# Pad lanes left out of the scatters, and two scatters of a block under way together, in an attention and mixture-of-experts kernel

## The chip, the cores and the metric

One core of one Trainium2 chip. The time is the device time of one execution in microseconds (us); lower is better. One execution was profiled. Its own time stands beside its span, which runs from the first to the last instruction.

## What is computed

The reference first computes attention with 4 batches, 8 heads, 576 positions and head size 64, with a bias on the scores made by a small network over relative positions. The result, read as 2304 rows of 512, is the input x of a mixture of 8 experts:

```python
logits = x @ w_gate
noise_scale = np.log1p(np.exp(x @ w_noise))
noisy_logits = logits + noise_scale * noise
top2 = np.argpartition(-noisy_logits, 2, axis=1)[:, :2]
...
out = np.zeros((N, D), dtype=np.float32)
for e in range(E):
    for k in range(2):
        mask = top2[:, k] == e
        h = np.maximum(x[mask] @ w1[e], 0.0)
        out[mask] += top2_w[mask, k, None] * (h @ w2[e])
```

Each row goes to two experts, so 4608 row visits are shared out. With the reference's inputs the experts get 616, 594, 556, 539, 534, 562, 609 and 598 of them.

## The kernel before, in words

**Stages.** The first stage, about 340 us, is the attention. During it the rows of x are stored to an HBM tensor (`xs`), and 128 pad rows of zeros are put behind them (L1592). The routing then makes lists of row numbers (`rowi`), one column per tile. The second stage is the experts.

**Blocks and tiles.** A block is up to 620 rows of one expert: 5 tiles (`BT`) of 124 rows (`ROWS`) each. A tile of indices has 128 lanes, and the lanes that hold no row of the expert hold a pad index, 2304 (`N`) or more, different in each lane. Here 8 blocks run, one for each expert: block 0 is written out by hand, then a hardware loop of 3 pairs of blocks, then a last block. The parity i says which of two sets of buffers a block uses (1 for odd blocks).

**One block.** POOL (GpSimd) gathers the rows of x by index into `xg` (L1620), ahead by one to two blocks, and the routing weights of the rows into `wrow` (L1625). PE transposes the rows (`xtr`, L773 to L780), ACT and DVE make a high and a low part of them (L1500, `xlow` L1258), and PE multiplies by the first weights (`first`, L782) and the second (`second`, L789), each in three passes. The second product of a tile lands in one of two banks `po`. DVE (in block 0 also ACT, `scaled0` at L1455 to L1458) multiplies it by the routing weight into one of two buffers `ys` (L1291, L1122). POOL then issues a scatter: an indirect DMA that adds the 128 rows of `ys` to the rows of the output that the indices name (L1633). A pad lane adds its row into one of 128 spare rows behind the output. The output was zeroed during the attention.

**What orders the work around the change.** One semaphore, `y_added`, counts the landings of the scatters and of the store of the pad rows, 16 for each DMA (`C_ADD` is the store's part). Waiting on it are:
- POOL in `scatter` (L1630): scatter g is issued once all g earlier ones have landed, and once its `ys` is there (L1631).
- POOL at the top of `block_of` (L1644), before it copies the block's indices into `iscat`, which the scatters read.
- DVE before it writes `ys` (L1290, L1121), and ACT before the third tile of block 0 (L1523): the scatter that read this buffer two tiles ago must have landed.
- POOL before the first gathers (L1667), for the store of the pad rows, and SP at the end (L565).

POOL works through its list in order. In block 0 that is: gathers of tiles 3 and 4, scatter 0, two weight gathers, scatter 1, the gathers of block 1 (tiles 0 to 2), scatter 2, tiles 3 and 4, one gather of block 2, scatter 3, two gathers, scatter 4, two gathers (L1680 to L1700). In a later block it is: index copies, five weight gathers, then gather and scatter in turn for tiles 0 to 2, two scatters, two gathers (L1642 to L1663). SP loads the expert weights in pieces of 512 KB into `wraw` (L506 to L512). ACT and DVE split each piece into a high and a low part (L1371, L989) in an order written out with their other work. For block 1 this is at L1296 to L1307: the last four splits, then `scaled0(3)`, then `xlow` of tiles 5 to 7.

Of the kernel before, what the change touches and what calls it, by code (L numbers as in the profile page):

```python
# [24 lines left out]
P = 128  # L25
# [4 lines left out]
N, DM, NE, F = B * S, H * D, 8, 1024  # L30
# [20 lines left out]
BT = 5  # L51
# [117 lines left out]
def build(nc, qT, kT, v, rtab, pcol, rcp8, w1c, b1c, w2b, wg, noise, mw1, mw2, consts, out, xs):  # L169
    ctx = ExitStack()  # L170
    with ctx:
# [3 lines left out]
        def sem(name):  # L175
            return ctx.enter_context(nc.semaphore(name))
# [33 lines left out]
        zeros = tmp("zeros", [P, DM])  # L210
# [209 lines left out]
        y_done = sem("y_done")  # L420
        y_added = sem("y_added")
        icopied = sem("icopied")
# [12 lines left out]
        def piece_rows(g, i, bank):  # L435
# [4 lines left out]
                    bank[0:XT, 0:len(cs) * 4 * D].rearrange("p (c e) -> p c e", c=len(cs)))  # L440

        CONSTS = 16 * (2 * GQ + 2)
        CONSTS2 = 16 * 3

        C_XLO, C_HLO, C_Y, C_ADD = 2, 4, 2, 16

# [8 lines left out]
        def _(sp):  # L455
# [103 lines left out]
            pairs = sp.value_load(blocks[0:1, NBLK:NBLK + 1], min_val=NE // 2 - 1, max_val=NBLK // 2 - 1)  # L559
            with sp.Fori(0, pairs) as k:  # L560
                for i in range(2):
                    e = expert(2 * k + 2 + i)
                    sp.wait_ge(y_ready, BT * (2 * k + i + 1))
                    load_expert(i, e)
            sp.wait_ge(y_added, C_ADD + 16 * BT * (2 * pairs + 2))  # L565
            sp.sem_inc(sp_passed, 1)
# [347 lines left out]
        def _(dve):  # L914
# [140 lines left out]
            for t in range(TILES):  # L1055
# [14 lines left out]
                b, at = divmod(t - 1 - GLAG - (H - 1) * NU, H * NU)  # L1070
# [47 lines left out]
            def scaled0(t):  # L1118
                dve.wait_ge(y_ready, t + 1)
                dve.wait_ge(w_rows, 16 * BT)  # L1120
                dve.wait_ge(y_added, C_ADD + 16 * (t - 1))  # L1121
                V.tensor_scalar(ys[t % 2][:, :], po[:, t % 2, :], wrow[:, t, 0:1], None, ALU.mult).then_inc(y_done, 1)  # L1122
# [146 lines left out]

            def block_of(b, i, last):  # L1270
                e = dve.value_load(blocks[0:1, bass.ds(b, 1)], min_val=0, max_val=NE - 1)
                for n in range(C_HALVES):
                    half, f = divmod(n, CF)
                    cols = slice(half * HB, (half + 1) * HB)
                    dve.wait_ge(hhi_done, C_HALVES * b + n + 1)
                    V.scalar_tensor_tensor(out=hC[1][:, f, cols], in0=ps[n % 4 // 2][:, n % 2, 0:HB], scalar=0.0,  # L1276
                                           in1=hC[0][:, f, cols].bitcast(F32), op0=ALU.max, op1=ALU.subtract)\
                        .then_inc(hlo_done, 1)
                    if n in XLATE:
                        t = XLATE[n]  # L1280
                        xlow(BT * b + t, (i + t) % 2, t)
                for t in range(BT):
                    g = BT * b + t
                    if not last and 2 * t < NC:
                        for c in (2 * t, 2 * t + 1):
                            split(b + 1, 1 - i, c, c)
                    dve.wait_ge(y_ready, g + 1)
                    if t == 0:
                        dve.wait_ge(w_rows, 16 * BT * (b + 1))
                    dve.wait_ge(y_added, C_ADD + 16 * (g - 1))  # L1290
                    V.tensor_scalar(ys[(i + t) % 2][:, :], po[:, (i + t) % 2, :], wrow[:, t, bass.ds(e, 1)], None, ALU.mult)\  # L1291
                        .then_inc(y_done, 1)
                    if not last and t < XB:
                        xlow(g + BT, (i + 1 + t) % 2, t)
# [14 lines left out]
            with dve.Fori(0, pairs) as k:  # L1309
                block_of(2 * k + 1, 1, False)  # L1310
                block_of(2 * k + 2, 0, False)
            block_of(2 * pairs + 1, 1, True)


        @block.scalar
        def _(act):
# [205 lines left out]
            xcopy(4, 0, 4)  # L1522
            act.wait_ge(y_added, C_ADD + 16)  # L1523
            scaled0(2)
# [18 lines left out]
        def _(pool):  # L1543
# [37 lines left out]
            def list_constants():  # L1581
# [9 lines left out]
                nc.gpsimd.memset(rowi[:, NL:NL + BT], N).then_inc(consts_done, 1)  # L1591
                pool.dma_start(xs[N:N + P, :], zeros[:, :]).then_inc(y_added, 16)  # L1592

# [7 lines left out]
            for n in range(B * H):  # L1601
                ahead = n + 2 < B * H
# [26 lines left out]
            def scatter(g, index, i):  # L1629
                pool.wait_ge(y_added, C_ADD + 16 * g)  # L1630
                pool.wait_ge(y_done, C_Y + g + 1)  # L1631
                pool.sem_inc(pool_passed, 1)
                nc.gpsimd.indirect_dma_start(out=out, out_offset=bass.IndirectOffsetOnAxis(ap=index, axis=0),  # L1633
                                             in_=ys[i][:, :], in_offset=None, compute_op=ALU.add,
                                             bounds_check=N + P - 1, oob_is_err=True).then_inc(y_added, 16)

# [4 lines left out]

            def block_of(b, i, ahead):  # L1642

                pool.wait_ge(y_added, C_ADD + 16 * BT * b)  # L1644
                pool.sem_inc(pool_passed, 1)
# [19 lines left out]
            for half in range(2):  # L1665
                pool.wait_ge(x_stored[half], 16 * (B - 1))
            pool.wait_ge(y_added, C_ADD)  # L1667
            pool.wait_ge(consts_done, 6)
# [34 lines left out]
            with pool.Fori(0, pairs) as k:  # L1703
                block_of(2 * k + 1, 1, True)
                block_of(2 * k + 2, 0, True)
            block_of(2 * pairs + 1, 1, False)


# [53 lines left out]
```

## Time and profile before

| | before |
|---|---|
| median of 3 runs | 798.24 us (796.75 to 800.86) |
| the profiled execution | 798.18 us, span 796.0 us, mean granted TensorE clock 0.988 |
| busy: PE (matmul) | 759.8 us, 95% of the span |
| busy: DVE, ACT, POOL | 492.2, 393.1, 383.2 us |
| software DMA queue (POOL's) | 10720 packets, 22.72 MB |
| the scatters in POOL's time | 40, about 1.6 us each |

How to read it: PE, DVE, ACT, POOL and SP are the engines TensorE, VectorE, ScalarE, GpSimd and SyncE; PEld is PE's weight load. L784 is line 784 of the kernel. The busy time of a DMA that POOL issues is the time in which POOL writes its descriptors, not the transfer. The chain is followed back from the last instruction, at each step to what released it. Releasers are inferred from semaphore events, so the engine named in a row can be the wrong one where the wait was for several things.

### The profile page before, as it was taken

How to read it: one execution, taken by the hardware profiler on the slowest of the kernel's cores; microseconds unless marked ns; L12 is line 12 of the kernel's file. 1: busy time of each engine (PE TensorE's matmuls, PEld its weight loads, DVE VectorE, ACT ScalarE, POOL GpSimd, SP SyncE). 2: the span in 40 equal slices, each digit the busy share in tenths (PEclk: the TensorE clock that was granted, in tenths of full speed). 3: DMA queues.
4: the chain of work that ended last, by engine and by line, in shares of the span. 5: the costliest groups of instructions: out<-in, count | busy, mean ns of one | idle time of the engine just before them, and what ended most of it. 6: DMA issues, size and time to landing. Idle time of an engine off the chain costs nothing.

```text
span 796.0 us, 18523 instructions
## 1 busy us (share of the span) xinstructions
PE 759.8 (95%) x6658; PEld 615.2 (77%) x6658; DVE 492.2 (62%) x1228; ACT 393.1 (49%) x843; POOL 383.2 (48%) x440
## 2 busy tenths in 40 slices
PE   4887999999999998999999999999999999999995
PEld 2335676776776765979898998998998988988984
DVE  6897999998999897886436235235344344354311
ACT  5996888888888786505334133233232232232200
POOL 0008999899899784035434324324424413423412
PEclk9998999999999999999999999999999999999998
DMA  7776343353353363319633724714804805713213
GB/s 165 211 232 150 112 134 104 103 164 103 100 166 99 95 203 148 86 26 297 194 137 66 203 77 75 234 35 79 264 6 76 263 12 81 251 26 66 41 19 48
DMA packets 51719, 98.49 MB, mean 124 GB/s; under 512 B 12736, under 2 KB 21696, under 8 KB 51648
## 3 DMA queue, kind: packets, MB, share of 16 engines
q1 hardware_dynamic: 40352, 74.55, 30.4%
q0 software_dynamic: 10720, 22.72, 14.5%
q8 instruction: 43, 0.70, 0.4%
q10 hardware_dynamic: 576, 0.29, 0.2%
q14 instruction: 28, 0.23, 0.1%
HBM read 66.38 MB, written 20.53 MB: 109 GB/s over the span
## 4 chain that ended last, share of the span: by engine, by line
PE 82%; DMA 6%; ACT 4%; DVE 3%; issue 3%; POOL 0%; POOLq 0%; SPq 0%; DVEq 0%; ACTq 0%
PE ps L784 26%; PE po L801 24%; PE po L696 11%; PE ps L614 8%; PE pt L641 6%; DMA slab<-work 2%; DMA out_rows<-ys,iscat 2%; PE pt L620 2%; ACT work L1331 2%; ACT work L1350 2%; PE pt L655 1%; PE pt L628 1%; DMA b1col<-in_b1c 1%; DVE ns L957 0%; DVE hT L1114 0%
## 5 line engine op out<-in xcount | busy, mean ns | idle before, releaser
L801 PE MATMUL po<-whi,hT 128*128 128x512 f32 (+1 forms) x640 | 162.7, 399 | 0.1
L784 PE MATMUL ps<-xT,whi 128*128 128x310 f32 (+1 forms) x960 | 160.0, 305 | 0.0
L1512 ACT ACTIVATE hT<-ps 128x310 fp32r<-128x310 f32 x112 | 48.2, 430 | 199.1 <-PE ps L784 199.1
L784 PEld LDWEIGHTS ps<-xT,whi 128*128 128x128 f32 x960 | 142.4, 189 | 0.9
L801 PEld LDWEIGHTS po<-whi,hT 128*128 128x128 f32 (+1 forms) x640 | 119.0, 189 | 26.0 <-DVE hT L1114 0.5
L1276 DVE SCALAR_TENSOR_TENSOR hT<-ps,hT 128x310 fp32r<-128x310 f32 x112 | 53.8, 481 | 133.2 <-ACT hT L1512 133.2
L1578 POOL TENSOR_SCALAR work<-work,rcp 128x576 f32<-128x576 f32 (+1 forms) x160 | 117.6, 745 | 25.6 <-DVE rcp L970 25.1
L1366 ACT ACTIVATE work<-ns,nmax 128x576 f32<-128x576 f32 (+1 forms) x160 | 123.1, 770 | 4.3 <-DVE nmax L957 4.2
L957 DVE CUSTOM_DVE_ANT_0 ns<-ps,slab 128x576 f32<-128x576 f32 (+1 forms) x160 | 119.7, 750 | 8.2 <-PE ps L614 6.4
L1620 POOL DMA_INDIRECT xg<-x_rows,igath x38 | 43.0, 1132 | 159.8 <-DVE ys L1291 74.2
L1633 POOL DMA_INDIRECT out_rows<-ys,iscat x35 | 60.3, 1724 | 95.1 <-DMA out_rows<-ys,iscat 65.1
L696 PE MATMUL po<-work,vs 128*64 128x288 f32 x640 | 98.2, 421 | 0.7 <-DVE xnat L985 0.7
L1291 DVE TENSOR_SCALAR ys<-po,wrow 128x512 f32<-128x512 f32 x35 | 26.3, 751 | 98.8 <-PE po L801 98.8
L784 PE MATMUL ps<-xT,wlo 128*128 128x310 f32 (+1 forms) x480 | 86.5, 302 | 0.0
L989 DVE TENSOR_TENSOR wlo<-wraw,whi 128x1024 fp32r<-128x1024 f32 x64 | 76.0, 1222 | 14.0 <-ACT whi L1371 14.0
L1381 ACT ACTIVATE work<-pt 128x320 f32<-128x320 f32 x144 | 62.9, 437 | 37.5 <-PE pt L641 30.6
L801 PE MATMUL po<-wlo,hT 128*128 128x512 f32 (+1 forms) x320 | 80.6, 394 | 0.0
L641 PEld LDWEIGHTS pt<-cst,work 64*128 64x128 f32 x1280 | 52.8, 141 | 35.1 <-POOL work L1578 19.4
L784 PEld LDWEIGHTS ps<-xT,wlo 128*128 128x128 f32 x480 | 72.8, 188 | 0.0
L801 PEld LDWEIGHTS po<-wlo,hT 128*128 128x128 f32 (+1 forms) x320 | 60.0, 188 | 14.2
L978 DVE COPY work<-pt 128x320 f32<-128x320 f32 x133 | 64.9, 488 | 9.9 <-PE pt L641 4.4
L641 PE MATMUL pt<-cst,work 64*128 64x64 f32 x1280 | 66.9, 231 | 2.8 <-DVE work L978 1.3
(181 smaller groups left out, 1109.0 us busy)
## 6 DMA issues: line engine op xcount, KB each, us to landing
wraw<-in_mw SPq DMA_DIRECT2D x64, 512.0 KB, 9.8
slab<-work SPq DMA_DIRECT2D x36, 288.0 KB, 3.7
qraw<-in_qT SPq DMA_DIRECT2D x64, 144.0 KB, 2.8
vs<-in_v SPq DMA_DIRECT2D x32, 160.0 KB, 2.5
out_rows<-zeros SPq DMA_DIRECT2D x32, 152.0 KB
kraw<-in_kT SPq DMA_DIRECT2D x64, 72.0 KB, 2.3
x_rows<-xnat SPq DMA_DIRECT2D x8, 576.0 KB, 4.3
xg<-x_rows,igath POOLq DMA_INDIRECT x38, 3.5
```

The costliest lines, as they stand in the source:

```text
L614: mm = nc.tensor.matmul(ps[t % 2][:, half, 0:HALF], qq[n % 2][part(half), u * P:(u + 1) * P], kk[n % 2][part(half), :], start=i == 0, stop ...
L641: mm = nc.tensor.transpose(pt[half][:, kt * D:(kt + 1) * D], E[t % ER][part(half), kt * P:(kt + 1) * P], ident[part(half), part(half)])
L696: mm = nc.tensor.matmul(po[half * D:(half + 1) * D, n % 2, 0:HALF], vs[n % 4][:, kt, :], PT[n % 2][:, kt, half * HALF:(half + 1) * HALF], ...
L784: mm = nc.tensor.matmul(ps[n % 4 // 2][:, n % 2, 0:w], w1s[i][pw][:, c, f * P:(f + 1) * P], x[px][:, c, :], start=j == 0 and c == 0, stop= ...
L801: mm = nc.tensor.matmul(po[0:m, (i + t) % 2, :], hT[px][:, at:at + m], w2s[i][pw][:, c, :], start=j == 0 and c == 0, stop=j == 2 and c == ...
L957: nc.vector.tensor_tensor_reduce(out=ns[t % 2][0:r, :].rearrange("p (a s) -> p a s", a=2), in0=ps[t % 2][0:r, :, 0:HALF], in1=bias[0:r, u, ...
L978: nc.vector.tensor_copy(PT[n % 2][:, :, u * P:u * P + D], pt[0][:, 0:NU * D].rearrange("p (k s) -> p k s", k=NU))\
L989: nc.vector.tensor_tensor(wlo[i][:, c * WC:(c + 1) * WC], wraw[i][:, c * WC:(c + 1) * WC], whi[i][:, c * WC:(c + 1) * WC].bitcast(F32), AL ...
L1366: nc.scalar.activation(E[t % ER][0:r, 0:S], ns[t % 2][0:r, :], ACT.Exp, bias=nmax[0:r, i:i + 1], scale=-1.0, accum_out=ssum[0:r, i:i + 1]) ...
L1381: nc.scalar.activation(PT[n % 2][:, :, at:at + D], pt[1][:, 0:NU * D].rearrange("p (k s) -> p k s", k=NU), ACT.Copy).then_inc(t_done[1], 1)
L1578: nc.gpsimd.tensor_scalar(E[t % ER][0:r, 0:S], E[t % ER][0:r, 0:S], rcp[0:r, i:i + 1], 1.0, ALU.mult, ALU.mult)\
L1633: nc.gpsimd.indirect_dma_start(out=out, out_offset=bass.IndirectOffsetOnAxis(ap=index, axis=0), in_=ys[i][:, :], in_offset=None, compute_o ...
```

## The change

Three things. The scatter's index check has the bound N - 1 in place of N + P - 1 and no longer counts an index beyond it as an error, so the lanes with pad indices are left out. `y_added` becomes two semaphores, one for each `ys` buffer (even and odd tiles), and the store of the pad rows gets its own. And `scatter` no longer waits for the earlier scatters: the wait before writing `ys` is for the last scatter of the same parity, and the top of `block_of` on POOL waits for all scatters of the block before, by two waits. `added(k, i, t)` gives 16 times the number of earlier tiles of the same parity.

```diff
-        y_added = sem("y_added")
+        y_added = [sem(f"y_added{i}") for i in range(2)]
+        xpad_stored = sem("xpad_stored")
...
+        def added(k, i, t):
+
+            return 16 * (BT * k + (BT * (2 - i) + t) // 2)
...
-            sp.wait_ge(y_added, C_ADD + 16 * BT * (2 * pairs + 2))
+            sp.wait_ge(y_added[0], 16 * BT * (pairs + 1))
+            sp.wait_ge(y_added[1], 16 * BT * (pairs + 1))
...
             def scaled0(t):
                 dve.wait_ge(y_ready, t + 1)
                 dve.wait_ge(w_rows, 16 * BT)
-                dve.wait_ge(y_added, C_ADD + 16 * (t - 1))
+                dve.wait_ge(y_added[t % 2], 16 * (t // 2))
...
-            def block_of(b, i, last):
+            def block_of(k, i, last):
+                b = 2 * k + 2 - i
...
-                    dve.wait_ge(y_added, C_ADD + 16 * (g - 1))
+                    dve.wait_ge(y_added[(i + t) % 2], added(k, i, t))
...
-            act.wait_ge(y_added, C_ADD + 16)
+            act.wait_ge(y_added[0], 16)
...
-                pool.dma_start(xs[N:N + P, :], zeros[:, :]).then_inc(y_added, 16)
+                pool.dma_start(xs[N:N + P, :], zeros[:, :]).then_inc(xpad_stored, 16)
...
             def scatter(g, index, i):
-                pool.wait_ge(y_added, C_ADD + 16 * g)
                 pool.wait_ge(y_done, C_Y + g + 1)
                 pool.sem_inc(pool_passed, 1)
                 nc.gpsimd.indirect_dma_start(out=out, out_offset=bass.IndirectOffsetOnAxis(ap=index, axis=0),
                                              in_=ys[i][:, :], in_offset=None, compute_op=ALU.add,
-                                             bounds_check=N + P - 1, oob_is_err=True).then_inc(y_added, 16)
+                                             bounds_check=N - 1, oob_is_err=False).then_inc(y_added[i], 16)
...
-            def block_of(b, i, ahead):
-
-                pool.wait_ge(y_added, C_ADD + 16 * BT * b)
+            def block_of(k, i, ahead):
+                b = 2 * k + 2 - i
+                for t in range(2):
+                    pool.wait_ge(y_added[(i + t) % 2], added(k, i, t))
...
-            pool.wait_ge(y_added, C_ADD)
+            pool.wait_ge(xpad_stored, 16)
```

The calls of `block_of` pass k in place of the block's number on DVE and POOL.

## Rows read from the trace of the kernel before

**Rows 1.** The page's part 4: shares of the chain by engine.

```profile
PE 82%; DMA 6%; ACT 4%; DVE 3%; issue 3%; POOL 0%; POOLq 0%; SPq 0%; DVEq 0%; ACTq 0%
```

**Rows 2.** Waits of PE from 335 us to the end: us in total, times, longest.

```profile
PE pt L620 <- issue: 2.0, 1, 2.0
PE pt L620 <- DMA xg<-x_rows,rowi: 0.3, 1, 0.3
```

**Rows 3.** The chain in order of time, 550 to 800 us: start, us, what.

```profile
702.66 5.57 PE po L801 x24
...
759.97 5.58 PE po L801 x24
...
765.88 0.76 DVE ys L1291
...
767.55 4.69 DMA out_rows<-ys,iscat
...
778.66 4.65 DMA out_rows<-ys,iscat
...
784.24 4.83 DMA out_rows<-ys,iscat
```

**Rows 4.** Timeline of the end: start, us, engine, line, operation, idle before.

```profile
788.06 0.75 DVE L1291 TENSOR_SCALAR ys<-po,wrow 128x512 f32<-128x512 f32 x1 [4.81 <-PE po L801]
790.00 1.55 POOL L1633 DMA_INDIRECT out_rows<-ys,iscat  x1 [4.21 <-DMA out_rows<-ys,iscat]
```

**Rows 5.** Windows at the end: busy time by engine, PE clock, DMA share, GB/s.

```profile
791.50:792.00 0.50, 0.00 (x0) 0.00 (x0) 0.00 (x0) 0.00 (x0) 0.06 (x1) 0.50 0.00 0
792.00:792.50 0.50, 0.00 (x0) 0.00 (x0) 0.00 (x0) 0.00 (x0) 0.00 (x0) 0.50 1.17 86
...
794.00:794.50 0.50, 0.00 (x0) 0.00 (x0) 0.00 (x0) 0.00 (x0) 0.00 (x0) 0.50 0.17 25
```

**Rows 6.** Waits of POOL from 596 to 653 us, one block.

```profile
POOL out_rows L1633 <- DMA out_rows<-ys,iscat: 8.2, 2, 4.3
```

**Rows 7.** Timeline of POOL in block 0.

```profile
360.14 1.02 POOL L1625 DMA_INDIRECT wrow<-w_rows,rowi  x1 [0.31 <-issue]
362.63 1.61 POOL L1633 DMA_INDIRECT out_rows<-ys,rowi  x1 [1.47 <-ACT ys L1458]
...
373.00 1.61 POOL L1633 DMA_INDIRECT out_rows<-ys,rowi  x1 [4.72 <-DMA out_rows<-ys,rowi]
```

**Rows 8.** Timeline of ACT in block 0.

```profile
351.07 0.69 ACT L1458 ACTIVATE ys<-po,wrow 128x512 f32<-128x512 f32 x1 [1.64 <-PE po L801]
...
361.72 0.69 ACT L1458 ACTIVATE ys<-po,wrow 128x512 f32<-128x512 f32 x1 [1.35 <-DMA wrow<-w_rows,rowi]
```

**Rows 9.** Timeline of all engines around PE's wait, 376 to 388 us.

```profile
377.86 2.11 PE L801 MATMUL po<-whi,hT 128*128 128x512 f32 x8
...
380.14 1.06 ACT L1371 ACTIVATE whi<-wraw 128x1024 fp32r<-128x1024 f32 x1 [1.07 <-DMA wraw<-in_mw]
...
381.24 1.23 DVE L989 TENSOR_TENSOR wlo<-wraw,whi 128x1024 fp32r<-128x1024 f32 x1 [0.90 <-ACT whi L1371]
...
383.04 1.25 DVE L1261 TENSOR_TENSOR xT<-pt,xT 128x496 fp32r<-128x496 f32 x2
...
383.81 0.61 PE L620 MATMUL pt<-cst,xg 124*128 124x124 f32 x4 [1.99 <-issue]
...
384.18 3.66 PE L801 MATMUL po<-whi,hT 128*128 128x512 f32 x8
```

**Rows 10.** Windows around the same wait; columns as in rows 5.

```profile
372.00:380.00 8.00, 8.00 (x40) 6.59 (x39) 4.91 (x5) 4.08 (x5) 5.50 (x5) 1.00 0.96 335
380.00:384.00 4.00, 2.01 (x10) 1.35 (x9) 3.10 (x5) 2.00 (x3) 1.24 (x1) 1.00 0.27 74
384.00:388.00 4.00, 4.00 (x15) 3.25 (x14) 1.09 (x3) 0.58 (x1) 3.36 (x3) 0.57 0.48 65
```

**Rows 11.** The scatters in POOL's time: ns, least, median and most.

```profile
L1633 POOL DMA_INDIRECT out_rows<-ys,iscat x35: 1552/1622/2159, 424.3 to 790.0; - x35
```

More of the change, by code:

```diff
@@ L440, in piece_rows @@
                     bank[0:XT, 0:len(cs) * 4 * D].rearrange("p (c e) -> p c e", c=len(cs)))
+        def added(k, i, t):
+            return 16 * (BT * k + (BT * (2 - i) + t) // 2)
         CONSTS = 16 * (2 * GQ + 2)
         CONSTS2 = 16 * 3
-        C_XLO, C_HLO, C_Y, C_ADD = 2, 4, 2, 16
+        C_XLO, C_HLO, C_Y = 2, 4, 2
         xw = nc.dram_tensor("w_rows", (N + P, NE), F32, kind="Internal").ap()
@@ L1309, in _ @@
             with dve.Fori(0, pairs) as k:
-                block_of(2 * k + 1, 1, False)
-                block_of(2 * k + 2, 0, False)
-            block_of(2 * pairs + 1, 1, True)
+                block_of(k, 1, False)
+                block_of(k, 0, False)
+            block_of(pairs, 1, True)
         @block.scalar
@@ L1703, in _ @@
             with pool.Fori(0, pairs) as k:
-                block_of(2 * k + 1, 1, True)
-                block_of(2 * k + 2, 0, True)
-            block_of(2 * pairs + 1, 1, False)
+                block_of(k, 1, True)
+                block_of(k, 0, True)
+            block_of(pairs, 1, False)
 def kernel(**inputs):
```

## The prediction

> **What bounds the kernel now.** I read the page's chain first, then the waits of TensorE, then the end of the chain in order of time, then the stretch in which the first scatters run. The page gives PE 82% of the chain and DMA 6% [rows 1]. In the list of waits from 335 us on, PE waits twice in 461 us: 2.0 us before a transpose of gathered rows, and 0.3 us [rows 2]. So from block 1 on PE runs without a gap, and a scatter can only matter where it holds that one wait of 2.0 us or stands behind PE's last instruction. In the last block the chain leaves PE at 765.55 and passes from scatter to scatter, each 4.5 to 4.8 us under way [rows 3]. That looks like a scatter-bound tail, but PE makes a tile in 5.57 us, and a scatter with its 0.93 us of queue steps takes 5.5 to 5.8 us: the two run level. What counts is the last tile. DVE ends the scaled rows of tile 4 at 788.06 + 0.75 = 788.81; the last scatter starts at 790.00 and waited for the one before, which had started at 784.24 and taken 4.83 us [rows 3, 4]. Its rows move between 792.0 and about 794.1, and the span ends at 796.0 [rows 5].
>
> **Part one: two scatters under way.** Before, scatter g waited for all earlier ones; now the landing is waited for by the engine that overwrites its buffer (ys), two tiles later, and by the next block's first scatter.
>
> Last scatter. Tile 0 of the last block shows the delay when nothing is under way: ys ends at 765.88 + 0.76 = 766.64, the scatter starts at 767.55, so 0.91 us [rows 3]. Tile 4 would start at 788.81 + 0.91 = 789.72 in place of 790.00: a gain of 0.28 us. All of it lies on the path that sets the end. ys of tile 4 itself needs scatter 2, landed at 778.66 + 4.65 = 783.31 [rows 3], which is long past.
>
> The six blocks in the middle. POOL loses waits of about 4 us before the scatters of tiles 3 and 4 (8.2 us in two waits in one block [rows 6]). They are worth nothing: PE has no wait there [rows 2]. The cover is the 57.3 us of PE work per block (702.66 to 759.97 [rows 3]). The fifth scatter of a block still waits for its own ys, so the copy of the next block's indices, behind all landings, moves by some tenths. The DVE wait is one against one, with a computed value in both versions.
>
> The first block. Scatter 0 had landed at about 361.70: ACT's ys of tile 2, which waits for that landing, starts at 361.72, and scatter 1 starts 0.93 us after it, at 362.63. The row names ACT ys as releaser, yet by the code scatter 1 needs ys of tile 1, which was done at 351.8; it was the landing [rows 7, 8]. Now scatter 1 can follow the weight gather that ends at 360.14 + 1.02 = 361.16, some 0.3 us later, at 361.46: 1.17 us earlier. Scatter 2 waited 4.72 us for scatter 1 [rows 7] and goes at about 368.6 in place of 373.00, and the two gathers queued behind it on POOL go some 4 us earlier too. Who gains? PE's wait of 2.0 us ends with DVE's subtraction for tile 5 (started 383.04). Before it in DVE's order stand ys of tile 3 and the last of the weight splits (381.24), which hangs on ACT (380.14), which waited 1.07 us for an expert weight load [rows 9]. So PE waits for the weight loads, and no scatter is in that chain except as a rival for the DMA engines. These are full: share 0.96 from 372 to 380, then 0.27 [rows 10]. Full engines do the same work in whatever order. Everything that I move ahead was also moved before 380 in the old order, so the last load ends when it did, less what the earlier start uses of free time before 363. The start is 1.17 us earlier, at the edge of the full stretch; I take 0.2 us off the wait, between 1.2 (the whole shift) and minus 4 (below, second rival).
>
> **Part two: pad lanes left out.** A tile has 124 real lanes of 128. The last tile of a block has fewer: the reference's inputs give the last expert 598 rows, so the last scatter carries 598 - 496 = 102 lanes, and 26 are left out. Its transfer takes 2.1 us [rows 5]. If time goes by bytes, that is 2.1 x 26/128 = 0.43 us less; if the engine with the most lanes decides and keeps its 8, nothing. Dealt round, the fullest engine would carry 7 lanes in place of 8: 0.26 us. I take 0.2, and both ends go into the range. The rows show the 16 engines evenly busy (share 1.17 falling to 0.17 in the last half microsecond), which tells nothing of how lanes are dealt. The Trainium skill ("DMA: Bandwidth & Descriptors", The descriptor swizzle) says that each engine carries eight fixed lanes in two runs of four, such as 64 to 67 and 96 to 99; lanes 102 to 127 would then leave some engines with all eight, and by it this term is 0 and my sum 0.2 us smaller. For other blocks the saved bytes (4 lanes a tile, up to 82 more in a last tile) are hidden behind PE.
>
> Leaving a lane out also changes what POOL does when it writes a scatter's descriptors: 1.55 to 2.16 us now [rows 11]. No row shows that form. Nearest are the scatters themselves; the cost lies between 0.6 less (one spread of these rows) and 0.6 more, and I take 0. It would count once, at the last scatter.
>
> **Small things.** The index copy waits for two semaphores in place of one, and so does SP at the end: all queue steps between ys and scatter together take 0.91 us [rows 3], so one more of them is put at 0.05 us on the path. The pad store has a semaphore of its own, with the same waiter.
>
> **Sum.** -0.28 (last scatter) -0.2 (lanes) -0.2 (PE's wait) +0.05 = -0.63 us. The profiled execution took 798.18 us (span 796.0 and 2.18 around it), so 797.55. The median of the runs shown, 798.24, stands 0.06 above it: 797.6.
>
> **The rivals.**
> One: PE's wait goes away. If the queue of scatters was slowing the weight loads more than by bytes, the last load lands 2 us earlier. Then PE gains the 2.0 us, and also the slow matmuls behind it: eight took 3.66 us after the pause, in a stretch whose granted clock was 0.57, near the 1.2 GHz level; eight of the same kind had taken 2.11 us before it [rows 9, 10]. That is 1.6 us more. With the tail's 0.43 it makes -4.0: 794.2, right at the edge of 0.5%. Against: full engines, and only 24 KB of pads left out of these three scatters. Chance 0.07, faster by over 0.5% in most of it.
> Two: the opposite. Scatter 2 and two gathers enter the queue earlier and push the loads back. Were none of these three served before the last load until now, they would cost it a scatter (about 2 us of transfer) and two gathers of about half that each: 4 us. PE's wait grows to 6.0 us: 798.2 + 4.0 - 0.43 = 801.8 at worst, and 799 to 800 for a part. Against: share 0.27 after 380 means that they were done by then. Chance 0.11, nearly all of it inside 0.5%.
> Three, on the other side: generating a scatter that may leave lanes out is much slower on POOL. Place: the tail, where scatter work and PE are level at 5.57 us. A scatter takes 1.55 + 0.9 us of POOL's time, so up to 3.1 us more fit into a tile's time, and only the last one's own excess counts. From there each tile adds to a lag. At 4.65 us more (four times now) POOL would take 7.1 us a tile: 4 x 1.5 + 4.65 = 10.7 later, 808.3 with the rest of the sum. It decides from about 3.4 us more on. For it: nothing in the rows shows the form. Against: the index check is there before as well. Chance 0.03.
> Four: leaving a lane out does not shorten anything, since each costs a descriptor all the same: -0.4, 797.8. Chance 0.24; it can hardly be told from the forecast.
>
> **How the numbers follow.** The forecast keeps 0.55. Everything but rivals one and three and the worst of two lies within 0.5% (4.0 us), about what a measurement of this kernel can tell from no change. Faster 0.06, same 0.90, slower 0.04. The range: unknown costs down (0.23 more by lanes, 0.6 by generation, 1.0 by the wait) give 795.8, up (rival two in part, 0.6 generation) about 800.5; the runs before spread by 4 us themselves. I give 795.3 to 800.6.
>
> **What would show it.** The last scatter starts 0.9 us after its ys and not after the landing before it. The wait of PE near 382 is 1.8 us. Scatter 1 starts near 361.5, scatter 2 near 368.6. No PE wait in the middle. Packets of the software queue fall by about 500 if a lane left out is not sent. I am wrong if PE's wait moves by over 1 us, if a scatter holds POOL for over 3 us, or if any block takes other than 57.3 us.

## The result, and the profile after

| | before | after |
|---|---|---|
| median of 12 runs | 797.68 us (795.86 to 800.86) | 800.12 us (796.73 to 803.70) |
| ratio, 95% interval | | 1.0034 [1.0020, 1.0048] |
| profiled execution | 798.18 us, span 796.0 | 800.05 us, span 798.2 |
| mean granted clock | 0.988 | 0.986 |

The changed kernel is slower, by 0.34% or 2.7 us (1.6 to 3.8). The forecast was 0.6 us faster; the time lies inside the range of 795.3 to 800.6, on the wrong side of no change.

The page's parts 2 to 4 of the changed kernel: packets in all, the software queue, shares of the chain by engine.

```profile
DMA packets 51720, 97.44 MB, mean 122 GB/s; under 512 B 13249, under 2 KB 22209, under 8 KB 51649
...
q0 software_dynamic: 10720, 21.67, 14.3%
...
PE 87%; ACT 3%; DMA 3%; DVE 3%; issue 2%; SPq 0%; POOLq 0%; POOL 0%; ACTq 0%; DVEq 0%
```

Against [rows 1] PE's share of the chain rose from 82% to 87% and DMA's fell from 6% to 3%: the scatters that stood in it one behind the other have left the chain, as meant. The queue still handles 10720 packets, for 1.05 MB less.

**The end.** The last tile in the changed kernel's timeline (to compare with [rows 4]), and the windows in which its rows move (to compare with [rows 5]).

```profile
790.45 0.75 DVE L1298 TENSOR_SCALAR ys<-po,wrow 128x512 f32<-128x512 f32 x1 [4.70 <-PE po L807]
...
792.07 1.55 POOL L1639 DMA_INDIRECT out_rows<-ys,iscat  x1 [3.90 <-DVE ys L1298]
```

```profile
793.50:794.00 0.50, 0.00 (x0) 0.00 (x0) 0.00 (x0) 0.00 (x0) 0.12 (x1) 0.50 0.00 0
794.00:794.50 0.50, 0.00 (x0) 0.00 (x0) 0.00 (x0) 0.00 (x0) 0.00 (x0) 0.50 1.22 66
...
796.00:796.50 0.50, 0.00 (x0) 0.00 (x0) 0.00 (x0) 0.00 (x0) 0.00 (x0) 0.50 0.25 41
```

The scatter starts 792.07 - 791.20 = 0.87 us after its rows are scaled, and what it waited for is DVE, not the landing. The rows still move for over 2 us, at 66 GB/s in the first window where it was 86. From issue to the end of the span it is 6.1 us, 6.0 before: 26 lanes fewer shortened nothing.

**The first block.** POOL's timeline (to compare with [rows 7]):

```profile
361.97 1.02 POOL L1632 DMA_INDIRECT wrow<-w_rows,rowi  x1 [0.31 <-issue]
363.29 1.61 POOL L1639 DMA_INDIRECT out_rows<-ys,rowi  x1 [0.30 <-issue]
366.80 1.07 POOL L1627 DMA_INDIRECT xg<-x_rows,rowi  x1 [1.90 <-DVE rowi L1098]
...
371.95 1.62 POOL L1639 DMA_INDIRECT out_rows<-ys,rowi  x1 [0.30 <-issue]
373.88 1.07 POOL L1627 DMA_INDIRECT xg<-x_rows,rowi  x1 [0.30 <-issue]
375.25 1.78 POOL L1627 DMA_INDIRECT xg<-x_rows,rowi  x1 [0.31 <-issue]
```

All of this block lies later on the clock than before, so the tables below count from one mark that the change doesn't reach, PE's transpose of tile 3: 357.60 before, 359.49 after. Counted so, scatter 1 starts at 3.80 in place of 5.03, and scatter 2 at 12.46 in place of 15.40, 2.9 us earlier, with its two gathers behind it. The forecast had scatter 2 4.4 us earlier; part of that was taken up by the gathers ahead of it, which end later than forecast. Now the wait of PE (to compare with [rows 9, 10]).

```profile
382.63 1.06 ACT L1378 ACTIVATE whi<-wraw 128x1024 fp32r<-128x1024 f32 x1 [1.42 <-DMA wraw<-in_mw]
...
383.73 1.23 DVE L995 TENSOR_TENSOR wlo<-wraw,whi 128x1024 fp32r<-128x1024 f32 x1 [1.25 <-ACT whi L1378]
...
386.30 0.61 PE L626 MATMUL pt<-cst,xg 124*128 124x124 f32 x4 [2.65 <-issue]
...
386.67 3.49 PE L807 MATMUL po<-whi,hT 128*128 128x512 f32 x8
```

```profile
376.00:380.00 4.00, 4.00 (x24) 3.35 (x23) 2.35 (x3) 1.75 (x2) 1.99 (x2) 1.00 1.06 342
380.00:382.00 2.00, 2.00 (x10) 1.64 (x9) 0.99 (x2) 1.06 (x1) 1.04 (x1) 1.00 0.64 258
...
386.70:390.10 3.40, 3.40 (x11) 2.68 (x10) 0.75 (x2) 0.58 (x1) 2.79 (x3) 0.54 0.43 39
```

The chain is the one the prediction read: a load of 512 KB, ACT's part, DVE's part, DVE's subtraction, PE. But the last load is used at 382.63 - 359.49 = 23.14 from the mark, where it was 380.14 - 357.60 = 22.54, and PE's wait grew from 1.99 to 2.65 us.

**The blocks between** (chain in order of time, to compare with the first lines of [rows 3]):

```profile
647.84 5.57 PE po L807 x24
...
705.16 5.57 PE po L807 x24
...
762.47 27.85 PE po L807 x120
```

57.32 and 57.31 us a block, as before. In the last block the chain stays with PE for all five tiles (120 matmuls), where it had left PE after the first.

So one profile of each kernel gives +1.9 us ahead of the mark, +0.6 from the mark to block 1's start (35.21 and 35.82) and -0.3 from there to the end: with one execution of each that settles nothing, as the spread over the runs below shows.

### The profile page after: what moved, and what is told of

It is laid out like the page before. It is cut to its first block, busy times and chain, and to the rows that moved or that the text cites. A ratio compares the mean times of both kernels' runs of the same rounds, so it can differ in the third digit from the quotient of the medians.

```text
span 798.2 us, 18492 instructions
## 1 busy us (share of the span) xinstructions
PE 762.2 (95%) x6658; PEld 617.5 (77%) x6658; DVE 491.8 (62%) x1228; ACT 393.8 (49%) x843; POOL 387.6 (49%) x440
## 3 DMA queue, kind: packets, MB, share of 16 engines
q0 software_dynamic: 10720, 21.67, 14.3%
## 4 chain that ended last, share of the span: by engine, by line
PE 87%; ACT 3%; DMA 3%; DVE 3%; issue 2%; SPq 0%; POOLq 0%; POOL 0%; ACTq 0%; DVEq 0%
PE po L807 28%; PE ps L790 26%; PE po L702 11%; PE ps L620 8%; PE pt L647 6%; DMA slab<-work 3%; PE pt L626 2%; ACT work L1338 2%; ACT work L1357 1%; PE pt L661 1%; PE pt L634 1%; DMA b1col<-in_b1c 1%; DVE wlo L995 1%; PE ps L596 1%; DVE hT L1120 0%
## 5 line engine op out<-in xcount | busy, mean ns | idle before, releaser
L1627 POOL DMA_INDIRECT xg<-x_rows,igath x38 | 41.3, 1087 | 178.3 <-DVE ys L1298 125.6
L1639 POOL DMA_INDIRECT out_rows<-ys,iscat x35 | 63.9, 1826 | 81.1 <-DVE ys L1298 75.2
L702 PE MATMUL po<-work,vs 128*64 128x288 f32 x640 | 100.2, 428 | 0.7 <-DVE xnat L991 0.7
L995 DVE TENSOR_TENSOR wlo<-wraw,whi 128x1024 fp32r<-128x1024 f32 x64 | 76.1, 1222 | 14.1 <-ACT whi L1378 11.4
```

Of the source, the lines that this page charges most:

```text
L702: mm = nc.tensor.matmul(po[half * D:(half + 1) * D, n % 2, 0:HALF], vs[n % 4][:, kt, :], PT[n % 2][:, kt, half * HALF:(half + 1) * HALF], ...
L995: nc.vector.tensor_tensor(wlo[i][:, c * WC:(c + 1) * WC], wraw[i][:, c * WC:(c + 1) * WC], whi[i][:, c * WC:(c + 1) * WC].bitcast(F32), AL ...
```

## The experiments

**Theories.** *Order of the transfers:* in block 0 the wait for scatter 1 had kept scatter 2 and two gathers back, so that they moved behind the weight loads; now they move ahead of them, the last load lands later and PE waits (the prediction's rival two). *DVE stopped by POOL:* in the changed kernel DVE stands still while POOL writes scatter 1's descriptors, and that delays the splits. *Lanes:* leaving lanes out costs something by itself. *Later blocks:* two scatters under way there disturb PE or its loads. The expectations were written before each set of runs and name the theories as they stood then: theory 1 and theory Q are the order of the transfers, theory 2 is the lanes, theory 3 is something outside the scatters, such as the attention stage or the program's code, and theory P is the stop of DVE.

All diffs are against the changed kernel, unless the kernel before is named. Ratios are against the kernel before on the same chip.

### First four: the parts alone

The lanes alone, on the kernel before (it still waits for every landing):

```diff
-                                             bounds_check=N + P - 1, oob_is_err=True).then_inc(y_added, 16)
+                                             bounds_check=N - 1, oob_is_err=False).then_inc(y_added, 16)
```

> Before's waits and its one semaphore, with only the index bound changed so that pad lanes are left out. Theory 1 (the loss comes from scatters of block 0 that enter the DMA queue earlier and hold back the weight loads): nothing of the order changes, so 0 to -0.4 us against before (797.3 to 797.7), and PE's wait near 382 us stays at about 2.0 us. Theory 2 (leaving lanes out is itself dearer, in descriptor writing or in transfer): the whole +2.4 us is here, about 800. Theory 3 (the loss has nothing to do with scatters, but with how the program's code or timing falls in the attention stage and in instruction fetches): the time differs from before by anything up to 2 us and the difference shows ahead of 340 us.

Block 0 one at a time, later blocks as changed (the five calls in block 0 pass `True`):

```diff
-            def scatter(g, index, i):
+            def scatter(g, index, i, serial=False):
+                if serial and g:
+                    pool.wait_ge(y_added[1 - i], 16 * ((g + 1) // 2))
```

> The changed kernel, but in block 0 each scatter again waits for the one before it; later blocks keep two under way, lanes are left out. Theory 1: the loss goes away, about 797.3, PE's wait back at 2.0 us, and DVE does not stop for 2 us before the last list of rows. Theories 2 and 3: stays at about 800.

Block 0 as changed, later blocks one at a time:

```diff
             def block_of(k, i, ahead):
...
+                    pool.wait_ge(y_added[(i + t + 1) % 2], 16 * (BT * k + (BT * (2 - i) + t + 1) // 2))
```

> The changed kernel, but in all blocks after block 0 each scatter again waits for the one before it. Theory 1: stays slow, about 800.4 (0.3 us of the last scatter given back). Theory 3: anything. If the time falls to about 798, the loss was in the later blocks, where neither profile shows a wait of PE.

And the changed kernel unaltered, as a repeat:

> The changed kernel once more, unaltered, for a second profile and more times: about 800. Theory 1: PE's wait near 384 us is 2.5 us or more again, and POOL's gathers of block 1 start at about 366.8 again. Theory 3: the 2 us of DVE before the last list of rows, or the 1.8 us that were lost ahead of 345 us, are not there or are elsewhere.

| | us | before | ratio [95%] |
|---|---|---|---|
| lanes alone | 797.45 | 798.05 | 0.9996 [0.9973, 1.0019] |
| block 0 one at a time | 796.08 | 798.05 | 0.9977 [0.9962, 0.9991] |
| later one at a time | 801.21 | 798.05 | 1.0038 [1.0020, 1.0056] |
| changed, again | 799.48 | 798.05 | 1.0014 [0.9996, 1.0031] |

This separates the two halves. With two under way in the later blocks alone the kernel is 2.0 us faster than before; with two under way in block 0 alone it is 3.2 us slower. The loss is in block 0, and the later blocks hide a gain under it. The lanes alone move nothing that can be measured. Two under way without leaving lanes out wasn't tried: two scatters would then add into the same spare rows at once.

The lanes' parts in detail. Scatters on POOL by line, of the lanes alone and then of the changed kernel (columns: busy us, mean ns, idle before):

```profile
L1633 POOL DMA_INDIRECT out_rows<-ys,iscat x35 | 59.9, 1712 | 98.0 <-DMA out_rows<-ys,iscat 67.6 <-DVE ys L1291 17.1 <-issue 13.3
```

```profile
L1639 POOL DMA_INDIRECT out_rows<-ys,iscat x35 | 63.9, 1826 | 81.1 <-DVE ys L1298 75.2 <-issue 5.9
```

The same group of the kernel before has 60.3 us, 1724 ns. So writing descriptors with lanes left out costs POOL nothing more, and rival three is out; having another scatter under way costs 0.1 us each, off PE's path. In the lanes' kernel the chain at the end reads:

```profile
764.92 4.82 DMA out_rows<-ys,iscat
...
770.72 4.92 DMA out_rows<-ys,iscat
...
776.56 5.01 DMA out_rows<-ys,iscat
...
782.50 4.96 DMA out_rows<-ys,iscat
```

4.8 to 5.0 us to a landing, where the kernel before had 4.5 to 4.8 in both its profiles. That is not the price of the lanes: a later variant of the kernel before ("before, held" below), which leaves no lane out, has 4.85 to 4.97 in the same four rows. The landings spread from 4.5 to 5.0 us in either form. With 0.9 us of queue steps the cycle is 5.8 to 5.9 us here against PE's 5.57 a tile, so a lag builds up from tile to tile. Its last scatter:

```profile
785.44 0.75 DVE L1291 TENSOR_SCALAR ys<-po,wrow 128x512 f32<-128x512 f32 x1 [4.80 <-PE po L801]
...
788.38 1.55 POOL L1633 DMA_INDIRECT out_rows<-ys,iscat  x1 [4.33 <-DMA out_rows<-ys,iscat]
```

It starts 2.19 us after its rows are scaled, against 0.87 in the changed kernel.

### Three that shift block 0's queue a little

If DVE's stop were the price, issuing scatter 1 after the routing list's last steps would remove it:

```diff
-            scatter(1, rowi[:, 1:2], 1)
             pool.wait_ge(routed_all, 1)
+            scatter(1, rowi[:, 1:2], 1)
```

> The changed kernel with one wait moved: POOL waits for the finished list of rows (routed_all) ahead of scatter 1 and not behind it, so its descriptors are written once DVE has made the list. Two scatters stay under way everywhere, and no scatter waits for another. Theory P (in the changed kernel DVE's first step of the list, a tensor_scalar, cannot start while POOL writes the descriptors of scatter 1, stops for 1.7 to 2.0 us, and the gathers and weight loads behind the list start late): DVE's stop is gone, POOL's gathers of block 1 start near 364.5 less what scatter 1 is later, PE's wait is back at 1.2 to 2.0 us, and the time is 796 to 797. Theory Q (it is scatter 2 and its gathers, 4 us earlier, that hold back the weight loads on full DMA engines): stays at 799.5 to 800.

Only scatter 1 waits, for scatter 0:

```diff
+            pool.wait_ge(y_added[0], 16)
             scatter(1, rowi[:, 1:2], 1)
```

> The changed kernel, but scatter 1 alone waits for scatter 0, as before the change; all others go without. Theory P: as f1, 796 to 797, since scatter 1 starts behind the list again. Theory Q: 799.5 to 800, since scatter 2 still goes early.

Only scatter 2 waits, for scatter 1:

```diff
+                    pool.wait_ge(y_added[1], 16)
                     scatter(2, rowi[:, 2:3], 0)
```

> The changed kernel, but scatter 2 alone waits for scatter 1, as before the change. Theory P: DVE's stop of 1.7 to 2.0 us stays, and so does the time, 799 to 800. Theory Q: back to 796 to 797.

Both waits, the kernel from the first four once more:

> The kernel of e3 once more, unaltered. It settles two things: whether 796.1 repeats (both theories: 796 to 797), and whether the twenty matmuls of attention near 314 us, which took 2.65 us in the profiles of the kernel before, e1 and e3 and 4.33 us at a lower clock in the three profiles of the changed kernel and e4, go with the program or with chance. If with the program, 2.65 us here and 4.33 us in f3; if with chance, either in each.

| | us | before | ratio [95%] |
|---|---|---|---|
| scatter 1 after the list | 799.65 | 798.39 | 1.0014 [0.9993, 1.0034] |
| scatter 1 waits | 798.47 | 798.39 | 1.0000 [0.9982, 1.0019] |
| scatter 2 waits | 798.57 | 798.39 | 1.0002 [0.9987, 1.0018] |
| both wait | 795.93 | 798.39 | 0.9975 [0.9958, 0.9992] |

The kernel with both waits repeats to 0.02%. Either wait alone gives back only part, and neither theory expected these times: the order had scatter 2 waiting at 796 to 797 and scatter 1 waiting at 799.5 to 800. The second is a miss that stays open: in its profile scatter 2 starts earliest of all and the load is used as late as in the changed kernel (table below), yet its time is level with the kernel before. In the profile in which scatter 2 waits, scatter 1 had started 1.2 us earlier for want of its own wait, so scatter 2 went at 14.0 from the mark, not at the 15.4 of before, and the last load still came at 22.8. In the profile with scatter 1 after the list the DVE stop is gone, and yet it has the longest wait of PE of all. Its timeline:

```profile
370.72 1.62 POOL L1639 DMA_INDIRECT out_rows<-ys,rowi  x1 [0.30 <-issue]
...
383.74 1.06 ACT L1378 ACTIVATE whi<-wraw 128x1024 fp32r<-128x1024 f32 x1 [1.37 <-DMA wraw<-in_mw]
...
387.40 1.05 PE L626 MATMUL pt<-cst,xg 124*128 124x124 f32 x4 [4.35 <-issue]
```

There scatter 2 starts at 370.72 - 358.89 = 11.8 from the mark, and the last load is used at 24.9, the latest of all. The stop is not the price; the order may be. The kernel with both waits, on its repeat, has these rows in its timeline:

```profile
380.14 1.06 ACT L1378 ACTIVATE whi<-wraw 128x1024 fp32r<-128x1024 f32 x1 [0.20 <-DMA wraw<-in_mw]
...
383.80 0.61 PE L626 MATMUL pt<-cst,xg 124*128 124x124 f32 x4 [0.94 <-issue]
...
384.17 2.09 PE L807 MATMUL po<-whi,hT 128*128 128x512 f32 x8
```

### Four that hold scatter 2 behind the last load

The direct trial of the order: leave two scatters under way, but let scatter 2 wait for the last weight load of block 1.

```diff
+                    pool.wait_ge(w_loaded[1][W1C - 1], 16)
                     scatter(2, rowi[:, 2:3], 0)
```

> The changed kernel with one wait more: POOL holds scatter 2, and with it the two gathers behind it, until the last weight load of block 1 has landed. Scatter 1 still goes without waiting for scatter 0. Theory Q (the loss in block 0 is one of order on full DMA engines: scatter 2 and the two gathers, sent 4 us earlier, go ahead of the last weight loads, which are what PE waits for): the last load comes 21.5 to 22.5 us after the transpose of tile 3 and not 23.1 to 24.9, PE's wait falls to 0.9 to 2.0 us, and the time to 796 to 797. Theory P (DVE's stop in front of the list): the stop is there or not as in the changed kernel, and the time stays at 799 to 800.

The same line in the kernel with both waits:

> The kernel of e3 (block 0 one scatter at a time, later blocks two under way) with the same hold of scatter 2. Theory Q: no slower than e3, 795 to 796; PE's wait 0.9 to 1.2 us, and then no matmuls at the lower clock behind it, which is worth another 1.5 us. If the hold only repeats what the wait for scatter 1 does, the same as e3.

A wait in the same place that has long been met when POOL comes to it, for the length of POOL's code alone:

```diff
+                    pool.wait_ge(zero_done, 1)
                     scatter(2, rowi[:, 2:3], 0)
```

> The changed kernel with one wait on POOL that has long been met, ahead of scatter 2: no order changes, only the length of POOL's code. It tests whether the twenty matmuls of attention near 314 us, at the lower clock in three profiles of three with exactly the POOL code of the changed kernel there (the changed kernel twice, e4), and at the higher one in seven profiles of seven without, follow the code's layout: then 2.65 us here and a time 1.2 to 1.7 us under the changed kernel's, 798.3. If chance: as the changed kernel, 799.5 to 800.

And the kernel before unaltered, one execution for its profile:

> The kernel before, for a second profile of it. Theory Q: the last weight load comes 21.5 to 22.6 us after the transpose of tile 3, PE's wait is 0.9 to 2.0 us.

| | us | before | ratio [95%] |
|---|---|---|---|
| scatter 2 held | 795.64 | 798.20 | 0.9967 [0.9950, 0.9984] |
| both waits and held | 797.37 | 798.20 | 0.9993 [0.9973, 1.0014] |
| met wait | 799.44 | 798.20 | 1.0008 [0.9990, 1.0025] |

One wait added to the changed kernel turns it from 0.34% slower to 0.33% faster (0.14% slower and 0.15% faster in the repeats). The met wait is the control for it: the two kernels differ only in what POOL waits for ahead of scatter 2, and side by side on one chip they took 799.44 and 795.64 us, with intervals that don't meet. The held kernel's timeline of POOL, then of all engines around PE's wait, then the windows there:

```profile
361.68 1.61 POOL L1639 DMA_INDIRECT out_rows<-ys,rowi  x1 [0.30 <-issue]
...
379.82 1.65 POOL L1639 DMA_INDIRECT out_rows<-ys,rowi  x1 [9.71 <-DMA wraw<-in_mw]
```

```profile
378.92 1.06 ACT L1378 ACTIVATE whi<-wraw 128x1024 fp32r<-128x1024 f32 x1 [0.20 <-DMA wraw<-in_mw]
...
382.59 0.61 PE L626 MATMUL pt<-cst,xg 124*128 124x124 f32 x4 [0.36 <-issue]
...
382.96 2.09 PE L807 MATMUL po<-whi,hT 128*128 128x512 f32 x8
```

```profile
376.00:380.00 4.00, 4.00 (x24) 3.32 (x23) 2.87 (x3) 3.19 (x4) 0.18 (x1) 1.00 0.27 108
380.00:382.00 2.00, 2.00 (x10) 1.49 (x8) 1.98 (x3) 0.93 (x2) 1.70 (x2) 1.00 0.00 0
382.00:384.00 2.00, 1.64 (x10) 1.27 (x10) 1.21 (x3) 0.59 (x1) 1.69 (x2) 1.00 1.03 124
```

Counted from the mark, scatter 2 starts 9.4 us later than in the changed kernel, the load is used at 21.0 from the mark in place of 23.1, PE waits 0.36 us in place of 2.65, and the eight matmuls behind it take 2.09 us in place of 3.49. Before 380 the DMA engines have room now (share 0.27, where the changed kernel has 1.06); the scatter and its gathers move after 382, when nobody waits for them. The hold moves the scatter and the two gathers together, so which of the three costs the load its time isn't told apart.

### Three more, with the cause still open

The hold alone on the kernel before, to see whether it is a gain of its own or only gives back what the change took:

> The kernel before with the hold alone: scatter 2 and the two gathers behind it wait for the last weight load of block 1 as well as for scatter 1. If it is their place in the order on the DMA engines that counts, PE's wait falls to 1.2 us or less and the time to 796 to 797.5; if the wait for scatter 1 already did all of it, no change (798).

The two held kernels again:

> The kernel of g2 once more (two under way, scatter 2 held), unaltered: 795.6 again if the gain is real, with the last weight load 21 us after the transpose of tile 3.

> The kernel of g3 once more (block 0 one at a time, and the hold), unaltered: 795 to 796.5 if its 797.4 was the spread of runs, 797.4 again if one at a time costs something once scatter 2 is held, as when scatters 2, 3 and 4 queue up one behind the other.

| | us | before | ratio [95%] |
|---|---|---|---|
| before, scatter 2 held | 797.47 | 798.16 | 1.0003 [0.9984, 1.0023] |
| changed, scatter 2 held | 796.72 | 798.16 | 0.9985 [0.9970, 1.0000] |
| both waits and held | 795.55 | 798.16 | 0.9968 [0.9955, 0.9982] |

On the kernel before the hold gains nothing in the time, though in its profile the load is used at 21.35. The wait for scatter 1 had nearly done the same there. The kernels with block 0 mended lie at 0.9967 to 0.9993 and change places on repeat (1.1 and 1.8 us between two trials of one kernel), so holding by the load and waiting for landings are not told apart. All medians are below the kernel before, though one interval reaches above 1; the best two trials, by 2.6 us each, beat both kernels of this case.

### All profiles side by side

Times from the transpose of tile 3: scatter 2's start, ACT's use of the last load, and block 1's start (PE's first transpose inside its loop). Then PE's wait, the eight matmuls behind it, and the time from block 1's start to the end of the span.

| profile | scatter 2 | last load | block 1 | PE's wait | eight | to the end |
|---|---|---|---|---|---|---|
| before | 15.4 | 22.54 | 35.21 | 1.99 | 3.66 | 403.19 |
| before, again | 15.3 | 21.22 | 32.34 | 0.74 | 2.10 | 403.79 |
| lanes alone | 16.9 | 21.67 | 32.79 | 1.20 | 2.10 | 404.41 |
| both waits | 16.9 | 22.45 | 35.13 | 1.91 | 3.39 | 402.74 |
| both waits, again | 16.0 | 21.54 | 32.64 | 0.94 | 2.09 | 402.76 |
| changed | 12.5 | 23.14 | 35.82 | 2.65 | 3.49 | 402.89 |
| changed, again | 11.4 | 23.67 | 36.35 | 2.34 | 3.48 | 402.81 |
| later one at a time | 12.4 | 23.15 | 35.82 | 2.63 | 3.28 | 403.95 |
| scatter 1 after the list | 11.8 | 24.85 | 37.61 | 4.35 | 3.35 | 403.00 |
| scatter 1 waits | 10.9 | 23.12 | 35.83 | 2.64 | 3.66 | 402.79 |
| scatter 2 waits | 14.0 | 22.75 | 35.39 | 2.33 | 3.28 | 402.71 |
| met wait | 12.5 | 22.81 | 33.93 | 2.35 | 2.10 | 402.98 |
| held | 21.9 | 20.98 | 32.09 | 0.36 | 2.09 | 402.77 |
| held, again | 21.9 | 20.99 | 32.09 | 0.33 | 2.09 | 402.85 |
| both waits and held | 21.6 | | 31.86 | 0.24 | 2.10 | 402.90 |
| both waits and held, again | 22.7 | 21.81 | 32.92 | 1.21 | 2.09 | 402.90 |
| before, held | 22.3 | 21.35 | 32.45 | 0.79 | 2.09 | 404.20 |

The mean of "last load" is 21.9 in the first five, 23.4 in the next seven and 21.3 in the held ones (four of five have the row); of "block 1" 33.6, 35.8 and 32.3. Scatter 2's start parts the groups: 15.3 to 16.9, 10.9 to 14.0, 21.6 to 22.7. Inside a group it doesn't order the loads (10.9 goes with 23.12, 11.8 with 24.85); there something else decides, which these runs don't show.

The profiles and the times agree on the size. Six trials with later blocks as changed have neither both waits nor the hold (changed twice, scatter 1 after the list, scatter 1 waits, scatter 2 waits, met wait): ratios 1.0000 to 1.0034, mean 1.0012. Six have one of them or both: 0.9967 to 0.9993, mean 0.9978. Between the means lie 2.8 us; block 1 starts at 35.8 on average in the profiles of the first six and at 32.8 in those of the others, 3.0 us apart.

One more rival, a later issue of the loads by SP, does not account for it. SP issues the last four loads of block 1 only when the routing list is done, so a stop of DVE can delay their issue. Counted from the mark, the last one is issued at 8.36 in the changed kernel and at 7.06 in the kernel before; but it is at 7.96 and 8.12 in the held kernel, which uses the load earliest, and at 7.23 with scatter 2 waiting, whose load comes at 22.75.

## Why the prediction was wrong

**The step that failed** is the one on PE's wait: "Full engines do the same work in whatever order. Everything that I move ahead was also moved before 380 in the old order, so the last load ends when it did". It was put at -0.2 us. In the profiles the last load comes 23.4 - 21.9 = 1.5 us later, and block 1 starts 35.8 - 33.6 = 2.2 us later. What was wrong in it: equal work keeps the end of the whole queue, not the end of one member of it, and PE waits for one member. That scatter 2 and the gathers behind it were done by about 380 did not mean that they had taken nothing from the last load, nor that they would take no more when issued earlier. How their packets mixed with the load's no view here shows; that the place of these three in the queue moves the load's end is what the held kernel shows. The one profile of before misled here too: its load, at 22.54, is the latest of the five in its group, so "PE's wait of 2.0 us" was taken as the normal state where 0.74 and 1.20 occur as well, and a delay looked as if it had to be added on top of an already long wait.

**Rival two** (chance 0.11) is what happened, in part of its size: its bound of 4 us was for all three transfers. Its argument against, the share of 0.27 after 380, was the same error as in the failed step. The direct evidence is the held kernel beside the met wait: one wait, and load, wait and matmuls all return.

**The slow matmuls** were priced in rival one only, as a gain of 1.6 us if the wait went away. The same price runs the other way. After waits up to 1.21 us the eight took 2.09 or 2.10 us, in all eight profiles with such a wait; after waits of 1.91 us and more they took 3.28 to 3.66 in eight of nine. So a wait of that length costs a further 1.2 to 1.6. Six of the seven profiles with scatter 2 early had it, and two of the five of the first group: that is how a load 1.5 us later made block 1 2.2 us later.

**The last scatter** was right in its mechanism: it starts 0.87 us after its rows are scaled, forecast 0.91. The size was off. In the profiles shown the gain from block 1's start to the end is 403.19 - 402.89 = 0.30 us, just the forecast's 0.28. But over all profiles with later scatters one at a time it is 403.9 on average (403.19 to 404.41), and 402.8 for two under way (402.71 to 403.00): 1.1 us. The term was read from one execution that happened to have short landings. The prediction itself put a scatter's cycle at 5.5 to 5.8 us against PE's 5.57, and didn't ask what a cycle at the upper end does over four tiles. The spread went with it: two under way makes the tail steady to 0.3 us.

**The lanes**: nothing in place of -0.2; here rival four (0.24) holds. The packets did not fall by 500: 10720 before and after, and those under 512 B rose from 12736 to 13248 in the kernel with lanes alone, by 512. Each lane left out is still a small packet. The Trainium skill ("DMA: Bandwidth & Descriptors", The descriptor swizzle) says that each engine carries eight fixed lanes in two runs of four, so that leaving out the top 26 spares some engines and leaves others with all eight. The trace agrees as far as it goes: the end after issue is unchanged (6.0 and 6.1 us). A slip without weight: a last tile can leave out up to 86 lanes more, not 82 (534 - 496 = 38 of 124 are filled).

**Right:** no wait of PE in the later blocks, 57.3 us a block, scatter 1 1.2 us earlier, no slower descriptor writing, the added semaphore waits too small to see.

**The sum** of what the profiles show is +2.2 - 1.1 = +1.1 us; measured were +2.7 (1.6 to 3.8) and, in the repeat, +1.1 (-0.3 to 2.5). By the times of the halves it is +3.2 for block 0 and -2.0 for the rest, together +1.2. The first measurement leaves 1.6 us without a cause shown, 0.5 us by the lower end of its interval. One candidate lies ahead of the mark, which itself lies anywhere from 357.2 to 359.5 in the 17 profiles. Twenty matmuls of the attention, before any scatter, in the changed kernel's timeline, and the window around them:

```profile
315.21 4.33 PE L702 MATMUL po<-work,vs 128*64 128x288 f32 x20 [0.68 <-DVE xnat L991]
```

```profile
310.00:320.00 10.00, 8.85 (x85) 5.01 (x81) 5.68 (x17) 5.62 (x12) 4.41 (x3) 0.83 0.17 52
```

and in the kernel before:

```profile
314.30 2.65 PE L696 MATMUL po<-work,vs 128*64 128x288 f32 x20 [0.68 <-DVE xnat L985]
```

They are 1.7 us slower at a granted clock of 0.83 over the ten microseconds. This is in three profiles (changed, changed again, later one at a time), which share POOL's code of block 0, and in none of the 14 others. The met wait was to tell whether the code's length does it: its profile has 2.65 us, but that is one of its fastest executions (795.93, of 794.82 to 801.32), and its time, 799.44, is not better than the changed kernel's in the repeat. So whether these 1.7 us belong to the change or fell by chance stays open.

## What to carry to other kernels

A wait that looks like pure loss can be what keeps a low-priority transfer behind an urgent one; before removing it, list what is queued behind it and which loads are in flight at that time, and if the wait must go, put the order back by waiting on the urgent load itself. "The same work in another order" speaks for the end of the queue, not for the end of the one load that is waited for: here that load came 1.5 us later on DMA engines as busy as before. And where two rates run nearly level, here 5.57 us of PE against 5.4 to 5.9 of scatter, one profile shows one draw of the lag: read its spread over several executions before pricing it.

## What was not expected of the hardware

**DVE stands still until POOL's descriptor writing ends.** In the changed kernel's DVE timeline, with POOL's scatter 1 at 363.29 + 1.61 = 364.90:

```profile
362.25 0.68 DVE L1267 TENSOR_TENSOR xT<-pt,xT 128x496 fp32r<-128x496 f32 x1 [0.67 <-ACT xT L1507]
...
364.92 0.30 DVE L1092 TENSOR_SCALAR rpad<-ps,padz 128x75 f32<-128x75 f32 x1 [2.00 <-remote]
```

A tensor_scalar of 0.30 us starts 0.02 us after POOL has ended, with 2.00 us of idle time in front of it. The same operation waited 1.65 to 2.0 us in all six profiles in which scatter 1 falls on it. In the five others of them it starts 0.05 to 0.09 us before POOL's recorded end (363.28 and 363.37 in the repeat of the changed kernel), and POOL's recorded times are rough. In the eleven other profiles its idle time is 0.55 us at most.

The six ends that coincide speak for POOL as what holds DVE up; no run shows by what means. The Trainium skill ("SBUF — State Buffer", Who interferes with whom) has DVE and GpSimd share a port pair that the first to issue holds for its whole instruction while the other fully blocks, but lets a tensor_scalar take it only in the modes that use two ports, and says that outside these modes a DVE instruction with at most one SBUF input does not contend. This one reads its rows from PSUM (`ps`) and one value per lane from SBUF (`padz`). The course of the stop is like the first statement; if the operation runs outside those modes, which no run here shows, the second would have no stop where the trace has up to 2.00 us.

It costs nothing that shows on the path: the stop is in the held kernel, one of the two fastest, and absent from the one that is slowest in block 0 (scatter 1 after the list).

**The clock after a wait.** In the window from 386.70 to 390.10 of the changed kernel the granted clock is 0.54, near the lower level of 1.2 GHz, after PE had waited 2.65 us. After 0.94 us of waiting, in the repeat of the kernel with both waits, it is 1.00 over the same eight matmuls (2.09 us). The length of the wait does not settle it alone: in the met wait's profile they ran at 1.00 (2.10 us) after 2.35 us of waiting.
